# Turning the gated stage's x in 32x32 squares on VectorE instead of on TensorE

## The chip, the cores and the metric

The kernel runs on one core of one Trainium2 chip. The metric is the device time of one execution in microseconds; the kernel before takes 614.62 us (median of three runs).

## The reference

Three layers follow one another: a recurrent attention over 4 x 8 heads of 768 steps, a mixture of eight experts over its 3072 tokens of 384 features, and the gated layers. The change touches the last alone, where N is 3072, DM 384 and FM 1024:

```python
def _moe2_ref(x, w1, w2, w3, w_out) -> np.ndarray:
    a = x @ w1
    b = x @ w2
    h = a * b @ w3
    return (h @ w_out).astype(np.float32)
```

## The kernel before

The core's engines run their own instruction streams and meet at semaphores. The attention comes first (to about 120 us), then routing and the experts, whose output rows are scattered to `xbuf` in DRAM, then `gated_layers` from about 300 us on. The product w3 @ w_out is folded into one matrix `wf` ahead of it (`Fold`), with TensorE's last part of that work placed around the first block.

`gated_layers` cuts the 3072 tokens into NB = 6 blocks of TOK = 512 (NI = 4 tiles of 128 tokens). A block needs x with its features on the partitions: KD = 3 tiles of 128 features by 512 tokens. Each float32 operand is split into a part `hi` that float32r holds and the remainder `lo`, and a product is made of three matmuls, hi by hi, hi by lo and lo by hi.

- SyncE (`gx.load`, L1082) loads a block's 512 rows of `xbuf` into `x_in`, tokens on the partitions, in two transfers of 384 KB; `x_in` has two slots, in the memory of an expert's weights that are no longer needed. The loads of blocks 0 and 1 are issued at the end of the experts, when the last scatter has landed; load(n) waits for TensorE's transposes of block n-2 (semaphore `s_T`). Its queue also issues the stores of the output (L1472), in the order load(n+2), store(n).
- TensorE turns x by 12 transposes of 128x128 a block (`transposes`, L1496), 8 into the banks `p_ab[0]` and 4 into a bank of `p_ab[1]`, and those of block n+1 stand at the end of block n. Then, for each of the KF = 8 tiles f of 128 hidden features, come `gates(t, f)` (L1508; 18 matmuls of 128x512, for a and b) and `outputs(t, f - 1)` (L1523; 12 matmuls of 128x384 that accumulate in the banks `p_o`).
- ScalarE makes `xT_hi` from PSUM (L1573), and per f copies a to SBUF (L1565, `a_sb`) and splits g into `g_hi` (L1568).
- VectorE makes `xT_lo` from PSUM (L1595), and per f the product g = a * b (L1588, `g_sb`) and `g_lo` (L1590).
- At the end of a block both copy `p_o` to `o_sb` (`out_copy`, L1579 and L1601), and SyncE stores it.

The order is written out by hand, engine by engine; `rounds` unrolls the first and last two blocks and loops over the two in the middle. `gates(t, f)` waits for g of f-2 (its banks), `outputs(t, f)` for `g_lo` of f, `outputs(t, 0)` also for the output copies of the block before. At the end of a block TensorE's order is gates(7), eight transposes of the next block, outputs(6), four transposes, outputs(7), and then gates(0) and gates(1) of the next block with nothing between them.

Of the kernel before, what the change touches and what calls it, by code (L numbers as in the profile page):

```python
# [12 lines left out]
P = 128  # L13
# [19 lines left out]

LINE = 1024
FRONT = 128
TABLE_BYTES = 2656


# [1030 lines left out]
class GatedInputs:  # L1069
# [3 lines left out]
    def __init__(self, sem, w1_in, TOK, DM):  # L1073
        self.TOK = TOK
        self.x_in = [w1_in[:, :, :].rearrange("p k f -> p (k f)")[:, i * TOK // P * DM:(i + 1) * TOK // P * DM].rearrange("p (i d) -> p i d", d=DM)
                     for i in range(2)]
        self.s_x = [[sem(f"x{i}{h}") for h in range(2)] for i in range(2)]

    def load(self, sp, xbuf, slot, n):
        TOK = self.TOK  # L1080
        for h in range(2):
            sp.dma_start(self.x_in[slot][:, 2 * h:2 * h + 2, :],  # L1082
                         xbuf[bass.ds(n * TOK + h * TOK // 2, TOK // 2), :].rearrange("(i p) d -> p i d", p=P)).then_inc(self.s_x[slot][h], 16)


def experts(nc, env, w1, w2, xbuf):
# [9 lines left out]
    with ExitStack() as ctx:  # L1096
# [74 lines left out]
        @block.sync  # L1171
        def _(sp):
            def load_w1(t, e=None):
                wait(sp, s_w1lo, t.num(NG, 0))
                ex.load_w1(sp, t.num() if e is None else e)

            def load_w2(t, e=None):
                wait(sp, s_w2lo, t.num(NG, 0))
                ex.load_w2(sp, t.num() if e is None else e)
            def load_wm(t):  # L1180
                if wm_block(t):
                    return
                wait(sp, fold.s_T, fold.KF)
                wait(sp, s_wmlo, t.num(1, -1))
                sp.dma_start(fold.w3_in[t.slot][:, :], wm[t.slot][bass.ds(t.turn(P), P), :]).then_inc(s_wmin[t.slot], 16)
            n = count_over(sp)
            sp.wait_ge(s_x[0], 32)
            rounds(sp, whole(sp, (load_wm, 0), (load_w1, 1), (load_w2, 1)), 2, E, 0, 0)

            def body(t, o):  # L1190
                e = sp.value_load(env["over_expert"][0:1, bass.ds(o, 1)], min_val=0, max_val=E - 1)
                load_w1(t, e)
                load_w2(t, e)
            overflow(sp, body, n)
            sp.wait_ge(s_w1lo, E * NG)
            sp.wait_ge(s_over, 1)
            for s in s_out:
                sp.wait_ge(s, 32 * env["n_scattered"])
            for i in range(2):
                env["gated_x"].load(sp, xbuf, i, i)  # L1200

        @block.gpsimd
        def _(pool):
# [207 lines left out]
def gated_layers(nc, env, xbuf, out):  # L1411
# [7 lines left out]
    with ExitStack() as ctx:  # L1419
# [3 lines left out]
        def sem(name):  # L1423
            return ctx.enter_context(nc.semaphore("gl_" + name))
# [9 lines left out]
        g_lo = [sb(f"g_lo{i}", [P, TOK], F32R) for i in range(2)]  # L1434
        o_sb = [sb(f"o_sb{i}", [P, NI, DM]) for i in range(2)]
        gx = env["gated_x"]
        x_in, s_x = gx.x_in, gx.s_x
        s_T, s_xhi, s_xlo = sem("T"), sem("xhi"), sem("xlo")
        s_ab, s_a, s_g, s_ghi, s_glo = sem("ab"), sem("a"), sem("g"), sem("ghi"), sem("glo")
        s_gout, s_o, s_oact, s_odve = sem("gout"), sem("o"), sem("oact"), sem("odve")  # L1440
        s_st = [sem(f"st{i}") for i in range(2)]
# [17 lines left out]
        with nc.Block() as block:  # L1459
            @block.sync  # L1460
            def _(sp):
                def load(t):
                    if isinstance(t.c, int) and t.num() < 2:
                        return
                    wait(sp, s_T, t.num(2, -2))
                    gx.load(sp, xbuf, t.slot, t.num())

                def store(t):
                    for h in range(2):
                        wait(sp, s_oact, t.num(2, h + 1))  # L1470
                        wait(sp, s_odve, t.num(2, h + 1))
                        sp.dma_start(out[bass.ds(t.num(TOK, h * TOK // 2), TOK // 2), :].rearrange("(i p) d -> p i d", p=P),  # L1472
                                     o_sb[t.slot][:, 2 * h:2 * h + 2, :]).then_inc(s_st[t.slot], 16)
                rounds(sp, whole((load, 2), (store, 0)), 2, NB, 2, 0)
                for i in range(2):
                    sp.wait_ge(s_st[i], 32 * NB // 2)
# [8 lines left out]
            def _(pe):  # L1485
                fold.product(pe, KF - 1, p_o[-1], (2,))
                pe.wait_ge(env["s_wmlo"], 2 * KD)

                def transposes(t, part):

                    wait(pe, s_g, t.num(KF, part - 1))
                    for i in range(NI):
                        if part == 0 and i % 2 == 0:
                            wait(pe, s_x[t.slot][i // 2], t.turn(16, 16))
                        for k in ((0, 1), (2,))[part]:
                            m = pe.transpose(p_ab[part][k % 2][:, i * P:(i + 1) * P], x_in[t.slot][:, i, k * P:(k + 1) * P], ident[:, :])  # L1496
                    m.then_inc(s_T, 1)

                def gates(t, f):
                    if f >= 2:  # L1500
                        wait(pe, s_g, t.num(KF, f - 1))
                    cols = slice(f * P, (f + 1) * P)
                    for w in range(2):
                        for k in range(KD):
# [22 lines left out]
                    m.then_inc(s_gout, 1)  # L1527

                def step(c, j):
                    t, nxt = Item(c, j, 0, 2), Item(c, j, 1, 2)  # L1530
                    if t.inside(NB):
                        for f in range(KF):
                            gates(t, f)
                            if f == KF - 1 and nxt.inside(NB):
                                transposes(nxt, 0)
                            if f:
                                outputs(t, f - 1)
                    if nxt.inside(NB):
                        if not t.inside(NB):
                            transposes(nxt, 0)  # L1540
                        transposes(nxt, 1)
                        if not t.inside(NB):
                            fold.product(pe, KF - 1, p_o[-1], (3,))
                    if t.inside(NB):
                        outputs(t, KF - 1)
                rounds(pe, step, 2, NB, 1, 0)

            @block.scalar
            def _(act):
# [1 line left out]
                    act.wait_ge(fold.s_Wout, f + 1)  # L1551
                    act.activation(wf_hi[:, f, :], fold.wf[:, f, :], ACT.Copy).then_inc(s_wfhi, 1)

                def wf_parts(t):

                    if isinstance(t.num(), int) and t.num() == 0:
                        for f in range(KF):
                            if f == KF - 1:
                                fold.taken(act, f, p_o[-1])
                            wf_part(f)  # L1560

                def products(t):
                    for f in range(KF):
                        wait(act, s_ab, t.num(KF, f + 1))
                        act.activation(a_sb[f % 2][:, :], p_ab[f % 2][0][:, :], ACT.Copy).then_inc(s_a, 1)  # L1565
                        wait(act, s_g, t.num(KF, f + 1))
                        wait(act, s_gout, t.num(KF, f - 1))
                        act.activation(g_hi[f % 2][:, :], g_sb[f % 2][:, :], ACT.Copy).then_inc(s_ghi, 1)  # L1568

                def x_hi(t):  # L1570
                    for k in range(KD):
                        wait(act, s_T, t.num(2, 1 + k // 2))
                        act.activation(xT_hi[t.slot][:, k, :], p_ab[k // 2][k % 2][:, :], ACT.Copy).then_inc(s_xhi, 1)  # L1573

                def out_copy(t):
                    wait(act, s_st[t.slot], t.turn(32))
                    for i in range(0, NI, 2):
                        first_or_all(act, t, i)
                        act.activation(o_sb[t.slot][:, i, :], p_o[i][:, 0:DM], ACT.Copy).then_inc(s_oact, 1)  # L1579
                rounds(act, whole((products, 0), (x_hi, 1), (wf_parts, 1), (out_copy, 0)), 2, NB, 1, 0)  # L1580

            @block.vector
            def _(dve):
                def products(t):
                    for f in range(KF):
                        wait(dve, s_a, t.num(KF, f + 1))
                        wait(dve, s_glo, t.num(KF, f - 1))
                        dve.tensor_tensor(g_sb[f % 2][:, :], a_sb[f % 2][:, :], p_ab[f % 2][1][:, :], ALU.mult).then_inc(s_g, 1)  # L1588
                        wait(dve, s_ghi, t.num(KF, f + 1))
                        dve.tensor_tensor(g_lo[f % 2][:, :], g_sb[f % 2][:, :], g_hi[f % 2][:, :], ALU.subtract).then_inc(s_glo, 1)  # L1590

                def x_lo(t):
                    for k in range(KD):
                        wait(dve, s_xhi, t.num(KD, k + 1))
                        dve.tensor_tensor(xT_lo[t.slot][:, k, :], p_ab[k // 2][k % 2][:, :], xT_hi[t.slot][:, k, :], ALU.subtract).then_inc(s_xlo, 1)  # L1595

                def out_copy(t):
                    wait(dve, s_st[t.slot], t.turn(32))
                    for i in range(1, NI, 2):
                        first_or_all(dve, t, i)  # L1600
                        dve.tensor_copy(o_sb[t.slot][:, i, :], p_o[i][:, 0:DM]).then_inc(s_odve, 1)  # L1601
                rounds(dve, whole((products, 0), (x_lo, 1), (out_copy, 0)), 2, NB, 1, 0)


def program(nc, r, k, v, w, u, moe_w_skip, moe_w_gate, moe_w1, moe_w2, moe2_w1, moe2_w2, moe2_w3, moe2_w_out, out):
# [83 lines left out]
```

## Time and profile before

| | us |
|---|---|
| median of three runs | 614.62 (613.81 to 615.62) |
| span of the profiled execution | 612.5 |
| around the span, against the median | 2.1 |
| TensorE busy in it | 595.1 (97%) |
| VectorE, ScalarE, GpSimd busy | 286.4, 228.1, 156.5 |

The profiled execution has no time of its own beside its span; the difference of 2.1 us to the median stands for what lies around it. A span goes from the first to the last instruction. PE is TensorE's matmuls, PEld its weight loads, DVE VectorE, ACT ScalarE, POOL GpSimd, SP SyncE, and SPq the transfers that it issues. PEclk is the clock that TensorE was granted, as a share of its full speed. Matmuls are pipelined, so that their recorded durations overlap: what one costs is read from the distance to the next start.

### The profile page before, as it was taken

How to read it: one execution, taken by the hardware profiler on the slowest of the kernel's cores; microseconds unless marked ns; L12 is line 12 of the kernel's file. 1: busy time of each engine (PE TensorE's matmuls, PEld its weight loads, DVE VectorE, ACT ScalarE, POOL GpSimd, SP SyncE). 2: the span in 40 equal slices, each digit the busy share in tenths (PEclk: the TensorE clock that was granted, in tenths of full speed). 3: DMA queues.
4: the chain of work that ended last, by engine and by line, in shares of the span. 5: the costliest groups of instructions: out<-in, count | busy, mean ns of one | idle time of the engine just before them, and what ended most of it. 6: DMA issues, size and time to landing. Idle time of an engine off the chain costs nothing.

```text
span 612.5 us, 17307 instructions
## 1 busy us (share of the span) xinstructions
PE 595.1 (97%) x7355; PEld 532.3 (87%) x7355; DVE 286.4 (47%) x459; ACT 228.1 (37%) x410; POOL 156.5 (26%) x179
## 2 busy tenths in 40 slices
PE   6699999999999999999999999999999999999997
PEld 6699999766999999999688888888898888888886
DVE  5489889283777777774121332232132133223212
ACT  3156666444665555552321222132132122213212
POOL 7568887215055544441230000000000000000000
PEclk9899999999999999999999999999999999999999
DMA  7779997596566777630400030020011001001001
GB/s 130 133 145 187 188 184 188 206 313 241 181 237 246 277 274 271 237 130 20 164 1 0 1 103 1 1 103 1 0 57 48 1 1 51 1 1 51 1 0 52
DMA packets 104258, 67.80 MB, mean 111 GB/s; under 512 B 79708, under 2 KB 98272, under 8 KB 104216
## 3 DMA queue, kind: packets, MB, share of 16 engines
q1 hardware_dynamic: 76360, 57.91, 30.8%
q10 hardware_dynamic: 25552, 4.72, 4.1%
q0 software_dynamic: 2304, 4.59, 2.3%
q8 instruction: 29, 0.48, 0.3%
q14 instruction: 13, 0.11, 0.1%
HBM read 55.92 MB, written 12.20 MB: 111 GB/s over the span
## 4 chain that ended last, share of the span: by engine, by line
PE 50%; DVE 0%; ACT 0%; issue 0%
PE gl_pab L1508 32%; PE gl_po L1523 8%; PE p_pair L1523 8%; PE gl_pab L1496 1%; PE p_pair L93 0%; DVE gl_g_lo L1590 0%; DVE gl_g_sb L1588 0%; ACT gl_g_hi L1568 0%; ACT gl_a_sb L1565 0%; DVE gl_o_sb L1601 0%
## 5 line engine op out<-in xcount | busy, mean ns | idle before, releaser
L1588 DVE TENSOR_TENSOR gl_g_sb<-gl_a_sb,gl_pab 128x512 f32<-128x512 f32 x48 | 33.0, 688 | 186.3 <-ACT gl_a_sb L1565 186.3
L1508 PE MATMUL gl_pab<-gl_xT_hi,wm_lo 128*128 128x512 f32 x288 | 112.9, 392 | 0.0
L1508 PE MATMUL gl_pab<-gl_xT_lo,wm_hi 128*128 128x512 f32 x288 | 112.8, 392 | 0.0
L1508 PE MATMUL gl_pab<-gl_xT_hi,wm_hi 128*128 128x512 f32 x288 | 112.1, 389 | 0.0
L1565 ACT ACTIVATE gl_a_sb<-gl_pab 128x512 f32<-128x512 f32 x48 | 28.8, 599 | 183.9 <-PE gl_pab L1508 183.9
L1508 PEld LDWEIGHTS gl_pab<-gl_xT_hi,wm_lo 128*128 128x128 f32 x288 | 54.0, 188 | 11.4
L1508 PEld LDWEIGHTS gl_pab<-gl_xT_hi,wm_hi 128*128 128x128 f32 x288 | 54.1, 188 | 10.6 <-DVE gl_xT_lo L1595 0.3
L1508 PEld LDWEIGHTS gl_pab<-gl_xT_lo,wm_hi 128*128 128x128 f32 x288 | 54.0, 188 | 10.5
L1265 PE MATMUL ex_ph<-ex_xT_hi,ew_w_hi 128*128 128x224 f32 x192 | 52.9, 275 | 0.0
L1265 PE MATMUL ex_ph<-ex_xT_hi,ew_w_lo 128*128 128x224 f32 x192 | 52.7, 274 | 0.0
L1265 PE MATMUL ex_ph<-ex_xT_lo,ew_w_hi 128*128 128x224 f32 x192 | 52.7, 274 | 0.0
L1590 DVE TENSOR_TENSOR gl_g_lo<-gl_g_sb,gl_g_hi 128x512 fp32r<-128x512 f32 x48 | 33.2, 692 | 33.5 <-ACT gl_g_hi L1568 33.5
L1568 ACT ACTIVATE gl_g_hi<-gl_g_sb 128x512 fp32r<-128x512 f32 x48 | 30.3, 632 | 36.2 <-DVE gl_g_sb L1588 36.2
L1281 PE MATMUL p_pair<-ew_w_hi,ex_h_hi 128*96 128x384 f32 (+1 forms) x128 | 43.4, 339 | 0.0
L1281 PE MATMUL p_pair<-ew_w_hi,ex_h_lo 128*96 128x384 f32 (+1 forms) x128 | 43.0, 336 | 0.0
L1281 PE MATMUL p_pair<-ew_w_lo,ex_h_hi 128*96 128x384 f32 (+1 forms) x128 | 43.0, 336 | 0.0
L1042 POOL DMA_INDIRECT ew_x_in<-xbuf,slot_token x16 | 22.5, 1406 | 71.3 <-DVE ex_x_new L1392 50.3
L93 PE MATMUL p_pair<-wo,w3T 128*128 128x384 f32 x112 | 38.8, 489 | 0.5 <-PEq L1652 0.4
L1265 PEld LDWEIGHTS ex_ph<-ex_xT_hi,ew_w_hi 128*128 128x128 f32 x192 | 36.8, 192 | 0.2
L1265 PEld LDWEIGHTS ex_ph<-ex_xT_lo,ew_w_hi 128*128 128x128 f32 x192 | 36.8, 192 | 0.1
L1265 PEld LDWEIGHTS ex_ph<-ex_xT_hi,ew_w_lo 128*128 128x128 f32 x192 | 36.9, 192 | 0.0
L1523 PE MATMUL gl_po<-gl_wf_hi,gl_g_hi 128*128 128x384 f32 x96 | 33.5, 349 | 0.7 <-DVE gl_g_lo L1590 0.7
(197 smaller groups left out, 1223.3 us busy)
## 6 DMA issues: line engine op xcount, KB each, us to landing
w_in<-in_moe_w SPq DMA_DIRECT2D x8, 1536.0 KB
ew_w_in<-in_moe_w SPq DMA_DIRECT2D x8, 1536.0 KB
w_in<-in_moe_w SPq DMA_DIRECT2D x14, 512.0 KB, 9.4
k_in<-in_k SPq DMA_DIRECT2D x48, 96.0 KB
v_in<-in_v ACTq DMA_DIRECT2D x48, 96.0 KB, 3.5
r_in<-in_r SPq DMA_DIRECT2D x48, 96.0 KB
w_in<-xbuf SPq DMA_DIRECT2D x12, 384.0 KB, 4.1
out<-gl_o_sb SPq DMA_DIRECT2D x12, 384.0 KB, 2.4
```

Of the source, the lines that this page charges most:

```text
L93: m = pe.matmul(bank[:, 0:self.DM], self.w3T[i % 3][:, g, :], self.wo[:, g, :], start=(g == 0), stop=(g == self.KF - 1), skip_group_check= ...
L1042: pool.indirect_dma_start(self.x_in[slot][0:tokens.shape[0], i, :], None, xbuf[:, :], bass.IndirectOffsetOnAxis(ap=tokens, axis=0), bounds ...
L1265: m = pe.matmul(p_h[g][:, f % 2, 0:width(t)], a[:, k, cols], b[:, k, 0:width(t)], start=(k == 0 and n == 0), stop=(k == KD - 1 and n == 2))
L1281: m = pe.matmul(p_y[i][0:n_tok, 0:DM], a[:, f, cols], b[:, f, :], start=(f == 0 and n == 0), stop=(f == KF - 1 and n == 2))
L1496: m = pe.transpose(p_ab[part][k % 2][:, i * P:(i + 1) * P], x_in[t.slot][:, i, k * P:(k + 1) * P], ident[:, :])
L1508: m = pe.matmul(p_ab[f % 2][w][:, :], a[:, w * KD + k, cols], b[t.slot][:, k, :], start=(k == 0 and n == 0), stop=(k == KD - 1 and n == 2))
L1523: m = pe.matmul(p_o[i][:, 0:DM], a[f % 2][:, cols], b[:, f, :], start=(f == 0 and n == 0), stop=(f == KF - 1 and n == 2))
L1565: act.activation(a_sb[f % 2][:, :], p_ab[f % 2][0][:, :], ACT.Copy).then_inc(s_a, 1)
L1568: act.activation(g_hi[f % 2][:, :], g_sb[f % 2][:, :], ACT.Copy).then_inc(s_ghi, 1)
L1588: dve.tensor_tensor(g_sb[f % 2][:, :], a_sb[f % 2][:, :], p_ab[f % 2][1][:, :], ALU.mult).then_inc(s_g, 1)
L1590: dve.tensor_tensor(g_lo[f % 2][:, :], g_sb[f % 2][:, :], g_hi[f % 2][:, :], ALU.subtract).then_inc(s_glo, 1)
```

## The change

Block 0 is loaded and turned as before (`load_first`, `first_transposes`). For blocks 1 to 5, the load writes x into `x_quad`, a view of the same two slots, in twelve transfers. Partition quarter q takes, of each tile k of 128 features, the 32 features k * 128 + 32 q to + 31: on its partition t lie, for each group g of 32 tokens, the features of token 32 g + t. VectorE then turns the 32x32 squares of one k by one instruction (`x_turn`, 128x512) into a new tile `xT`, with the features on the partitions. x_hi and x_lo of these blocks read `xT` instead of PSUM. All this is done in the steps of the block before: x_turn(k) in f = 1 + k, x_hi(k) in f = 2 + k, x_lo(k) in f = 3 + k.

TensorE's transposes of blocks 1 to 5 go, and its order becomes one sequence over the blocks: gates(0) of the next block comes ahead of outputs(7) of the block before it, and the output copies come behind the product of f = 0 of the next block. load(n) for n over 2 waits for the turns of block n-2 (`s_turned`).

```diff
+        self.x_quad = [x.rearrange("p i d -> p (i d)").rearrange("p (g k e) -> p g k e", k=DM // P, e=QUAD) for x in self.x_in]
+        self.s_x = [sem(f"x{h}") for h in range(2)]
+        self.s_xq = [sem(f"xq{i}") for i in range(2)]
...
+    def load(self, sp, xbuf, slot, n):
+        TOK = self.TOK
+        rows = xbuf[bass.ds(n * TOK, TOK), :].rearrange("(g t) (k q e) -> q k t g e", t=QUAD, q=P // QUAD, e=QUAD)
+        for q in range(P // QUAD):
+            for k in range(self.x_quad[slot].shape[2]):
+                sp.dma_start(self.x_quad[slot][q * QUAD:(q + 1) * QUAD, :, k, :], rows[q, k]).then_inc(self.s_xq[slot], 16)
...
-            for i in range(2):
-                env["gated_x"].load(sp, xbuf, i, i)
+            env["gated_x"].load_first(sp, xbuf)
+            env["gated_x"].load(sp, xbuf, 1, 1)
...
+        xT = sb("xT", [P, KD, TOK])
+        NQ = 16 * KD * P // QUAD
+        s_T, s_turned, s_xhi, s_xlo = sem("T"), sem("turned"), sem("xhi"), sem("xlo")
...
-                    wait(sp, s_T, t.num(2, -2))
+                    if isinstance(t.c, int) and t.num() == 2:
+                        sp.wait_ge(s_T, 2)
+                    else:
+                        wait(sp, s_turned, t.num(KD, -2 * KD))
...
-                    if f >= 2:
-                        wait(pe, s_g, t.num(KF, f - 1))
+                    wait(pe, s_g, t.num(KF, f - 1))
...
-                    t, nxt = Item(c, j, 0, 2), Item(c, j, 1, 2)
-                    if t.inside(NB):
-                        for f in range(KF):
+                    t, before = Item(c, j, 0, 2), Item(c, j, -1, 2)
+                    for f in range(KF):
+                        if t.inside(NB):
                             gates(t, f)
-                            if f == KF - 1 and nxt.inside(NB):
-                                transposes(nxt, 0)
-                            if f:
+                        if f:
+                            if t.inside(NB):
                                 outputs(t, f - 1)
-                    if nxt.inside(NB):
-                        if not t.inside(NB):
-                            transposes(nxt, 0)
-                        transposes(nxt, 1)
-                        if not t.inside(NB):
-                            fold.product(pe, KF - 1, p_o[-1], (3,))
-                    if t.inside(NB):
-                        outputs(t, KF - 1)
-                rounds(pe, step, 2, NB, 1, 0)
+                        elif before.inside(NB):
+                            outputs(before, KF - 1)
+                first_transposes(0)
+                first_transposes(1)
+                fold.product(pe, KF - 1, p_o[-1], (3,))
+                rounds(pe, step, 2, NB, 0, 1)
...
+                def x_hi(t, k):
+                    wait(act, s_turned, t.num(KD, k + 1 - KD))
+                    act.activation(xT_hi[t.slot][:, k, :], xT[:, k, :], ACT.Copy).then_inc(s_xhi, 1)
...
+                def step(c, j):
+                    t, before, nxt = Item(c, j, 0, 2), Item(c, j, -1, 2), Item(c, j, 1, 2)
+                    for f in range(KF):
+                        if t.inside(NB):
+                            product(t, f)
+                        if f == 0 and before.inside(NB):
+                            out_copy(before)
+                        if 2 <= f < 2 + KD and nxt.inside(NB):
+                            x_hi(nxt, f - 2)
...
+                def x_turn(t, k):
+                    if k == 0:
+                        wait(dve, s_xq[t.slot], t.turn(NQ, NQ if t.slot else 0))
+                    wait(dve, s_xlo, t.num(KD, k + 1 - KD))
+                    dve.transpose(xT[:, k, :].rearrange("p (g e) -> p g e", e=QUAD), x_quad[t.slot][:, :, k, :]).then_inc(s_turned, 1)
+                def x_lo(t, k):
+                    wait(dve, s_xhi, t.num(KD, k + 1))
+                    dve.tensor_tensor(xT_lo[t.slot][:, k, :], xT[:, k, :], xT_hi[t.slot][:, k, :], ALU.subtract).then_inc(s_xlo, 1)
...
+                def step(c, j):
+                    t, before, nxt = Item(c, j, 0, 2), Item(c, j, -1, 2), Item(c, j, 1, 2)
+                    for f in range(KF):
+                        if t.inside(NB):
+                            product(t, f)
+                        if f == 0 and before.inside(NB):
+                            out_copy(before)
+                        if nxt.inside(NB):
+                            if 1 <= f < 1 + KD:
+                                x_turn(nxt, f - 1)
+                            if 3 <= f < 3 + KD:
+                                x_lo(nxt, f - 3)
```

## Rows read from the trace of the kernel before

**Rows 1.** The page's part 1: busy us (share of the span) and number of instructions.

```profile
PE 595.1 (97%) x7355; PEld 532.3 (87%) x7355; DVE 286.4 (47%) x459; ACT 228.1 (37%) x410; POOL 156.5 (26%) x179
```

**Rows 2.** Windows, one block each: busy us (instructions), granted clock, DMA share, GB/s.

```profile
455.90:507.00 51.10, 51.10 (x254) 45.11 (x253) 13.95 (x21) 12.40 (x21) 0.00 (x0) 1.00 0.10 32
507.00:558.00 51.00, 51.00 (x254) 45.01 (x253) 13.96 (x21) 12.40 (x21) 0.00 (x0) 1.00 0.04 16
```

**Rows 3.** The chain that ended last, in order of time (start, us, engine, line).

```profile
568.56 4.12 PE gl_pab L1508 x18
```

**Rows 4.** Windows of the transposes' line L1496 alone, one block.

```profile
404.80:455.90 51.10, 1.63 (x12) 1.43 (x12) 1.00 0.09 32
```

**Rows 5.** Timeline of ACT: start, us, line, tile, shapes, idle before it and releaser.

```profile
311.13 0.60 ACT L1565 ACTIVATE gl_a_sb<-gl_pab 128x512 f32<-128x512 f32 x1 [2.10 <-PE gl_pab L1508]
...
362.20 0.60 ACT L1565 ACTIVATE gl_a_sb<-gl_pab 128x512 f32<-128x512 f32 x1 [2.10 <-PE gl_pab L1508]
...
399.57 0.60 ACT L1565 ACTIVATE gl_a_sb<-gl_pab 128x512 f32<-128x512 f32 x1 [4.24 <-PE gl_pab L1508]
...
413.27 0.60 ACT L1565 ACTIVATE gl_a_sb<-gl_pab 128x512 f32<-128x512 f32 x1 [2.10 <-PE gl_pab L1508]
...
603.86 0.60 ACT L1565 ACTIVATE gl_a_sb<-gl_pab 128x512 f32<-128x512 f32 x1 [4.24 <-PE gl_pab L1508]
```

**Rows 6.** Timeline of PE at the end of block 1, and in block 5.

```profile
399.13 0.39 PE L1508 MATMUL gl_pab<-gl_xT_hi,wm_lo 128*128 128x512 f32 x1
...
400.16 0.42 PE L1523 MATMUL gl_po<-gl_wf_hi,gl_g_hi 128*128 128x384 f32 x1
...
402.18 0.34 PE L1523 MATMUL p_pair<-gl_wf_hi,gl_g_lo 128*128 128x384 f32 x1
...
402.70 0.42 PE L1523 MATMUL gl_po<-gl_wf_hi,gl_g_hi 128*128 128x384 f32 x1
...
597.20 0.39 PE L1508 MATMUL gl_pab<-gl_xT_hi,wm_lo 128*128 128x512 f32 x1
597.43 0.33 PE L1523 MATMUL gl_po<-gl_wf_hi,gl_g_hi 128*128 128x384 f32 x1
597.60 0.34 PE L1523 MATMUL gl_po<-gl_wf_lo,gl_g_hi 128*128 128x384 f32 x1
```

**Rows 7.** Timeline of DVE and PE in block 0, f=1 and 2.

```profile
313.15 0.69 DVE L1590 TENSOR_TENSOR gl_g_lo<-gl_g_sb,gl_g_hi 128x512 fp32r<-128x512 f32 x1 [0.70 <-ACT gl_g_hi L1568]
317.99 0.69 DVE L1588 TENSOR_TENSOR gl_g_sb<-gl_a_sb,gl_pab 128x512 f32<-128x512 f32 x1 [4.14 <-ACT gl_a_sb L1565]
319.37 0.69 DVE L1590 TENSOR_TENSOR gl_g_lo<-gl_g_sb,gl_g_hi 128x512 fp32r<-128x512 f32 x1 [0.70 <-ACT gl_g_hi L1568]
...
323.38 0.33 PE L1523 MATMUL gl_po<-gl_wf_hi,gl_g_hi 128*128 128x384 f32 x1
```

**Rows 8.** DVE: L1601 (ns min/median/max), L536 (busy us, mean ns); ACT: L1568 likewise.

```profile
L1601 DVE COPY gl_o_sb<-p_pair x6: 557/558/558, 354.0 to 609.0; 128x384 f32<-128x384 f32 x6
...
L536 DVE TENSOR_TENSOR w_sq<-w_sq 128x4 f32<-128x4 f32 x6 | 1.0, 161 | 0.2
...
L1568 ACT ACTIVATE gl_g_hi<-gl_g_sb 128x512 fp32r<-128x512 f32 x48 | 30.3, 632 | 36.2 <-DVE gl_g_sb L1588 36.2
```

**Rows 9.** DMA of 1 to 26 us by queue; issue durations of L262; landings, page part 6.

```profile
q1 hardware_dynamic: 14990, 2.79, 59.4%
...
L262 SPq DMA_DIRECT2D k_in<-in_k x48: 595/638/1684, 1.7 to 93.1; - x48
...
v_in<-in_v ACTq DMA_DIRECT2D x48, 96.0 KB, 3.5
...
w_in<-xbuf SPq DMA_DIRECT2D x12, 384.0 KB, 4.1
```

**Rows 10.** Timeline of SP's transfers and of PE at the stage's start.

```profile
294.74 7.76 SPq L1082 DMA_DIRECT2D w_in<-xbuf  x6
...
300.12 1.15 PE L1496 MATMUL gl_pab<-ident,w_in 128*128 128x128 f32 x9
```

More of the change, by code:

```diff
@@ L35 @@
 FRONT = 128
+QUAD = 32
 TABLE_BYTES = 2656
@@ L1076, in __init__, with load_first @@
                      for i in range(2)]
-        self.s_x = [[sem(f"x{i}{h}") for h in range(2)] for i in range(2)]
+        self.x_quad = [x.rearrange("p i d -> p (i d)").rearrange("p (g k e) -> p g k e", k=DM // P, e=QUAD) for x in self.x_in]
+        self.s_x = [sem(f"x{h}") for h in range(2)]
+        self.s_xq = [sem(f"xq{i}") for i in range(2)]
+    def load_first(self, sp, xbuf):
+        TOK = self.TOK
+        for h in range(2):
+            sp.dma_start(self.x_in[0][:, 2 * h:2 * h + 2, :],
+                         xbuf[h * TOK // 2:(h + 1) * TOK // 2, :].rearrange("(i p) d -> p i d", p=P)).then_inc(self.s_x[h], 16)
     def load(self, sp, xbuf, slot, n):
         TOK = self.TOK
-        for h in range(2):
-            sp.dma_start(self.x_in[slot][:, 2 * h:2 * h + 2, :],
-                         xbuf[bass.ds(n * TOK + h * TOK // 2, TOK // 2), :].rearrange("(i p) d -> p i d", p=P)).then_inc(self.s_x[slot][h], 16)
+        rows = xbuf[bass.ds(n * TOK, TOK), :].rearrange("(g t) (k q e) -> q k t g e", t=QUAD, q=P // QUAD, e=QUAD)
+        for q in range(P // QUAD):
+            for k in range(self.x_quad[slot].shape[2]):
+                sp.dma_start(self.x_quad[slot][q * QUAD:(q + 1) * QUAD, :, k, :], rows[q, k]).then_inc(self.s_xq[slot], 16)
 def experts(nc, env, w1, w2, xbuf):
@@ L1436, in gated_layers @@
         gx = env["gated_x"]
-        x_in, s_x = gx.x_in, gx.s_x
-        s_T, s_xhi, s_xlo = sem("T"), sem("xhi"), sem("xlo")
+        x_in, s_x, x_quad, s_xq = gx.x_in, gx.s_x, gx.x_quad, gx.s_xq
+        xT = sb("xT", [P, KD, TOK])
+        NQ = 16 * KD * P // QUAD
+        s_T, s_turned, s_xhi, s_xlo = sem("T"), sem("turned"), sem("xhi"), sem("xlo")
         s_ab, s_a, s_g, s_ghi, s_glo = sem("ab"), sem("a"), sem("g"), sem("ghi"), sem("glo")
@@ L1487, in _, with first_transposes @@
                 pe.wait_ge(env["s_wmlo"], 2 * KD)
-                def transposes(t, part):
-                    wait(pe, s_g, t.num(KF, part - 1))
+                def first_transposes(part):
                     for i in range(NI):
                         if part == 0 and i % 2 == 0:
-                            wait(pe, s_x[t.slot][i // 2], t.turn(16, 16))
+                            pe.wait_ge(s_x[i // 2], 16)
                         for k in ((0, 1), (2,))[part]:
-                            m = pe.transpose(p_ab[part][k % 2][:, i * P:(i + 1) * P], x_in[t.slot][:, i, k * P:(k + 1) * P], ident[:, :])
+                            m = pe.transpose(p_ab[part][k % 2][:, i * P:(i + 1) * P], x_in[0][:, i, k * P:(k + 1) * P], ident[:, :])
                     m.then_inc(s_T, 1)
                 def gates(t, f):
-                    if f >= 2:
-                        wait(pe, s_g, t.num(KF, f - 1))
+                    wait(pe, s_g, t.num(KF, f - 1))
                     cols = slice(f * P, (f + 1) * P)
@@ L1552, in wf_part, with wf_parts, product, first_x_hi @@
                     act.activation(wf_hi[:, f, :], fold.wf[:, f, :], ACT.Copy).then_inc(s_wfhi, 1)
[L1554 to L1562, printed above, removed]
-                    for f in range(KF):
[L1564 to L1570, printed above, removed]
-                    for k in range(KD):
-                        wait(act, s_T, t.num(2, 1 + k // 2))
-                        act.activation(xT_hi[t.slot][:, k, :], p_ab[k // 2][k % 2][:, :], ACT.Copy).then_inc(s_xhi, 1)
+                def wf_parts():
+                    for f in range(KF):
+                        if f == KF - 1:
+                            fold.taken(act, f, p_o[-1])
+                        wf_part(f)
+                def product(t, f):
+                    wait(act, s_ab, t.num(KF, f + 1))
+                    act.activation(a_sb[f % 2][:, :], p_ab[f % 2][0][:, :], ACT.Copy).then_inc(s_a, 1)
+                    wait(act, s_g, t.num(KF, f + 1))
+                    wait(act, s_gout, t.num(KF, f - 1))
+                    act.activation(g_hi[f % 2][:, :], g_sb[f % 2][:, :], ACT.Copy).then_inc(s_ghi, 1)
+                def first_x_hi():
+                    for k in range(KD):
+                        act.wait_ge(s_T, 1 + k // 2)
+                        act.activation(xT_hi[0][:, k, :], p_ab[k // 2][k % 2][:, :], ACT.Copy).then_inc(s_xhi, 1)
+                def x_hi(t, k):
+                    wait(act, s_turned, t.num(KD, k + 1 - KD))
+                    act.activation(xT_hi[t.slot][:, k, :], xT[:, k, :], ACT.Copy).then_inc(s_xhi, 1)
                 def out_copy(t):
@@ L1579, in out_copy @@
                         act.activation(o_sb[t.slot][:, i, :], p_o[i][:, 0:DM], ACT.Copy).then_inc(s_oact, 1)
-                rounds(act, whole((products, 0), (x_hi, 1), (wf_parts, 1), (out_copy, 0)), 2, NB, 1, 0)
+                def step(c, j):
[7 more added lines that the diff above has]
+                            x_hi(nxt, f - 2)
@@ L1582, in _ @@
+                first_x_hi()
+                wf_parts()
+                rounds(act, step, 2, NB, 0, 1)
             @block.vector
             def _(dve):
[L1584 to L1590, printed above, removed]
@@ L1592, in x_lo, with product @@
-                def x_lo(t):
-                    for k in range(KD):
-                        wait(dve, s_xhi, t.num(KD, k + 1))
-                        dve.tensor_tensor(xT_lo[t.slot][:, k, :], p_ab[k // 2][k % 2][:, :], xT_hi[t.slot][:, k, :], ALU.subtract).then_inc(s_xlo, 1)
+                def product(t, f):
+                    wait(dve, s_a, t.num(KF, f + 1))
+                    wait(dve, s_glo, t.num(KF, f - 1))
+                    dve.tensor_tensor(g_sb[f % 2][:, :], a_sb[f % 2][:, :], p_ab[f % 2][1][:, :], ALU.mult).then_inc(s_g, 1)
+                    wait(dve, s_ghi, t.num(KF, f + 1))
+                    dve.tensor_tensor(g_lo[f % 2][:, :], g_sb[f % 2][:, :], g_hi[f % 2][:, :], ALU.subtract).then_inc(s_glo, 1)
@@ new lines, in first_x_lo @@
+                def first_x_lo():
+                    for k in range(KD):
+                        dve.wait_ge(s_xhi, k + 1)
+                        dve.tensor_tensor(xT_lo[0][:, k, :], p_ab[k // 2][k % 2][:, :], xT_hi[0][:, k, :], ALU.subtract).then_inc(s_xlo, 1)
+                def x_turn(t, k):
[3 more added lines that the diff above has]
+                    dve.transpose(xT[:, k, :].rearrange("p (g e) -> p g e", e=QUAD), x_quad[t.slot][:, :, k, :]).then_inc(s_turned, 1)
@@ L1601, in out_copy @@
                         dve.tensor_copy(o_sb[t.slot][:, i, :], p_o[i][:, 0:DM]).then_inc(s_odve, 1)
-                rounds(dve, whole((products, 0), (x_lo, 1), (out_copy, 0)), 2, NB, 1, 0)
+                def step(c, j):
[10 more added lines that the diff above has]
+                                x_lo(nxt, f - 3)
+                first_x_lo()
+                rounds(dve, step, 2, NB, 0, 1)
 def program(nc, r, k, v, w, u, moe_w_skip, moe_w_gate, moe_w1, moe_w2, moe2_w1, moe2_w2, moe2_w3, moe2_w_out, out):
```

## Prediction

> **What bounds the kernel now.** I read the page's busy shares first: TensorE is busy for 97% of the span [rows 1], and the gated stage, which starts near 300 us [rows 10], is half of it. The reader is to see next that this stage has no other limit: cut into its six blocks, every window of a full block shows PE busy for its whole length at a granted clock of 1.00, with DVE at 14.0 us and ACT at 12.4 us of 51 [rows 2]. The chain of waits says the same: it runs through PE's matmuls, in pieces like the 18 of a gates group in 4.12 us [rows 3]. So an instruction of PE that goes away in blocks 0 to 4 is worth its whole slot, as long as nothing else becomes late; work moved to DVE costs nothing while it fits DVE's idle time. The slots are read from the starts of consecutive instructions, not from the durations, because the pipelined matmuls overlap: the 12 transposes of one block count as 1.63 us busy [rows 4], but take less, as follows.
>
> **What is removed: the transposes of blocks 1 to 5 on PE, 60 of them.** ScalarE starts each a_sb copy as soon as a gates group ends, so its starts are the clock of the stage. Inside a block, from f=1 to f=7, they are 399.57 - 362.20 = 37.37 us apart, 6.228 us per step (18 gates matmuls, 12 outputs matmuls) [rows 5]. From f=7 of one block to f=1 of the next it is 413.27 - 399.57 = 13.70 us, where two plain steps would be 12.46: the block boundary costs 1.24 us. After the change a boundary is a plain step: PE does gates(0) of the new block, then outputs(7) of the old one. Over the stage: from f=1 of block 0 (311.13) to f=7 of block 5 (603.86) is 292.73 us [rows 5]; there are 46 steps, and 46 x 6.228 = 286.49. **Saved: 6.24 us.** The other way to size it is the gap that the transposes open: last gates matmul to first outputs matmul 1.03 us with the first eight between them, 0.23 without; the last four sit in a gap of 0.52 us where 0.17 is usual [rows 6]. That is 0.80 + 0.35 = 1.15 us, and up to 0.09 more for each of the two outputs groups behind a transpose, whose first matmul lasts 0.42 us instead of 0.33: at most 1.33 us a block, 6.65 us in all. I take 6.24, since it is measured over the whole stage, with all that a boundary does to the matmuls around it, and keep 6.65 for the low end.
>
> **What is added on DVE: three turns of 128x512 a block**, in steps f=1 to 3, and x_lo in f=3 to 5. DVE is idle 4.14 us in front of the g_sb of a step [rows 7]. No row shows a 32x32 transpose. From below, a DVE copy of 384 columns is 0.56 us [rows 8]. From above, if each of the 16 squares of a row were paid like an instruction of its own, the row of a tiny DVE instruction, 0.161 us [rows 8], gives 2.6 us. I take 0.7, as a pass over 128x512 is 0.69 us [rows 7] and the number of elements is the same. The fullest step is f=3: one turn and one x_lo, 1.4 of 4.1 us. At 2.6 it still fits (3.3). Behind it stands a second cover: g_lo of f=2 is done at 319.37 + 0.69 = 320.06 and PE takes it up at 323.38, 3.3 us later [rows 7]. So PE waits only once three turns together pass 3 x 4.14 - 0.69 + 3.3 = 15.0 us, 5.0 each. Cost: nothing. The Trainium skill ("VectorE: DVE Perf Modes", The three transpose paths) sends a 128x128 transpose to TensorE, since DVE only turns 32x32 squares; here the load brings the quarters into place, and by that page's 311 ns for 128x128 in bf16 the turn would be an estimated four times that at most, 1.2 us, which changes nothing in the sum.
>
> **What moves on ACT and DVE.** The three x_hi and x_lo leave the boundary, where they read PSUM, and go into steps with 4.1 to 4.2 us idle; a pass over SBUF costs 0.63 us on ACT (g_hi) [rows 8] and 0.69 on DVE (g_lo) [rows 7]: nothing. x_hi(k) waits for a turn that was made a step earlier, and behind it on ACT stands only the next a_sb. The output copies now lie behind product(0) of the next block, and outputs(0), one gates group later, waits for them. With T the end of gates(0): g_lo ends at T + 2.7 (the distance from ACT's a_sb at 311.13 to the end of g_lo at 313.84), the two DVE copies of 0.56 us follow [rows 8] and end at T + 3.9; PE needs them at T + 6.2, a whole step later (outputs, 2.1, then gates, 4.1). Cover 2.3 us: nothing. If it failed it would cost PE its excess at each of five boundaries.
>
> **What moves on SP and the DMA queues.** A load was 2 issues of 384 KB and becomes 12 of 64 KB, 512 packets of 128 bytes each. The nearest rows are k_in and r_in: 96 KB, also 512 packets (192 bytes), 0.638 us an issue; and the queue that carried them moved 14990 packets in 25 us in 59.4% of 16 engines' time, 16 ns a packet [rows 9]. So 32 packets per engine take 0.5 us, less than the issue: SP sets the pace, 12 x 0.64 = 7.7 us a load. Block 0's own load keeps its form and goes first. Block 1's starts about 1 us after SP's first issue at 294.74 and is all issued by 303.5; with the 3.5 us from issue to landing of the v_in row [rows 9] it is there by 307. DVE asks for it after g_lo of f=1, at 313.84; 7 us to spare, and PE itself would not wait before 317.99 - 0.7 + 3.3 = 320.6 [rows 7, 10]. Block 2's load (303.5 to 311.2) has until block 1. Loads 3 to 5 come behind a store, as before, and in front of the next store, a block of 51 us later [rows 2]; each has over 40 us. A new wait stands on SP: load(n) on the turns of block n-2, made a whole block before. Cost: nothing. That loads don't slow PE shows in two blocks, one with a load under it (DMA share 0.10) and one without (0.04): PE does the same 254 matmuls in both in 51.1 and 51.0 us [rows 2].
>
> What stays: block 0's start, the fold, the last outputs, copies and stores. Block 0's load may land a little earlier or later now that smaller packets stand behind it: plus or minus 0.4 us, estimated from its 5.4 us between 294.74 and the transposes at 300.12 [rows 10].
>
> **Sum.** The profiled span is 612.5 us, and the runs' median 614.62, 2.1 us around it. Span after: 606.3; time: 614.62 - 6.24 = **608.4 us**.
>
> **Rivals.**
> (a) *Block 1's load lands too late, slower than before.* Transfers into a quarter of the partitions may be slower than into half. DVE then stands at x_turn with g_sb of f=2 behind it, ACT and PE follow. It begins to cost at 320.6, that is if each of the 12 transfers takes over (320.6 - 295.8)/12 = 2.1 us, 3.2 times the row's 0.64; it reaches slower than before at 2.6 us each. At 3 us, 295.8 + 36 = 332, a stall of 11: 620 us. Only the first load can, unless a load takes over 50 us. Against it: the rows' packets go to half of the partitions at 16 ns each, and the new ones keep 32 elements in order on both sides. Chance 0.04. The Trainium skill ("VectorE: DVE Perf Modes", The three transpose paths) speaks for this rival: a plain copy that transposes by its strides is 19 times slower than one through the crossbar. By it a load would take an estimated 19 x 4.1 us [rows 9] = 78 us, over a block, all five would bound, and the time would pass 680 us; no row shows such a copy. The same notes speak against it ("SBUF — State Buffer", Door 1: The DMA port swizzle): a range of 32 partitions reaches as many ports as one of 64.
> (b) *A turn over 5 us.* Each us above it costs PE 3 us a block, 15 us in all; slower than before from 5.4 us. Three turns of 6 us: 608.4 + 15 = 623. For it: no row shows the operation. Against: even 16 separate instructions stay below, at 2.6 us. Chance 0.02.
> (c) *The gain is given back at the boundary:* outputs(0) waits for the output copies, or gates(1) for the last g. The rows leave 2.3 us of cover, so it would take an order on ACT or DVE that I misread. With 1.2 us of wait per boundary: 614.4, no change. Chance 0.05.
> (d) *PE's pace falls,* because DVE, ACT and DMA now read and write beside matmuls at more places. 0.5% of 292 us is 1.5: 609.9; against it stand the equal blocks of [rows 2]. Chance 0.05.
> Forecast as it stands, 0.84.
>
> **How the numbers follow.** Low: lowest run 613.81 - 6.65 - 0.4 = 606.8. High: highest run 615.62 - 6.24 = 609.4, plus one unseen wait of 0.4 us at each of five boundaries, 611.4; that takes in (d). About 0.3%, 1.8 us, is what a measurement of this kernel can tell from no change. Faster: forecast and most of (d), 0.89. Same: (c) and the rest, 0.05. Slower: (a) and (b), 0.06.
>
> **What would show it.** In the profile after: 12 PE transposes instead of 72, all ahead of block 0; a_sb starts 6.23 us apart across the boundaries too; no PE idle with DVE as its releaser; a DVE group of 15 turns near 0.7 us; DVE's wait in front of the first turn empty; the load's issues near 0.64 us. I would be wrong if PE shows idle time near 314 to 330 us (a), DVE fills its steps (b), PE waits at the boundaries (c), or a step is longer than 6.23 us (d).

## Result and profile after

The changed kernel takes 616.42 us (median of 20 runs, 613.97 to 618.61) against 615.05 us for the kernel before in the same comparison: a ratio of 1.0021, 95% interval 1.0012 to 1.0030. It is slower by 0.2%, where 608.4 us were forecast. The profiled execution is the fastest of the 20, 613.97 us with a span of 612.2, which is 0.3 us under the span of the kernel before (612.5).

The page's part 1 of the kernel after, to be held against [rows 1]: the sixty transposes are gone (7355 to 7295 PE instructions), DVE has 15 more.

```profile
PE 590.4 (96%) x7295; PEld 526.9 (86%) x7295; DVE 294.7 (48%) x474; ACT 227.0 (37%) x410; POOL 156.4 (26%) x179
```

Inside the stage everything went as forecast. The timeline of ACT after, f=1 of block 0 and f=7 of block 5, answers to [rows 5]; under it the durations of the turns (min/median/max, ns):

```profile
317.12 0.60 ACT L1575 ACTIVATE gl_a_sb<-gl_pab 128x512 f32<-128x512 f32 x1 [2.09 <-PE gl_pab L1524]
...
603.55 0.60 ACT L1575 ACTIVATE gl_a_sb<-gl_pab 128x512 f32<-128x512 f32 x1 [4.24 <-PE gl_pab L1524]
...
L1627 DVE STREAM_TRANSPOSE gl_xT<-w_in x15: 703/705/705, 319.7 to 531.5; 128x512 f32<-128x512 f32 x15
```

286.43 us lie between the two copies, 6.30 less than before; forecast were 286.49 and 6.24. A turn costs 0.70 us. But the first line stands at 317.12 where it stood at 311.13: the stage begins 6.0 us later. The timelines of SP and PE after show where, beside [rows 10]:

```profile
294.99 0.93 SPq L1086 DMA_DIRECT2D w_in<-xbuf  x2
295.97 6.85 SPq L1096 DMA_DIRECT2D w_in<-xbuf  x12
...
295.86 2.74 PE L94 MATMUL p_pair<-wo,w3T 128*128 128x384 f32 x8
...
303.35 2.90 PE L94 MATMUL p_pair<-wo,w3T 128*128 128x384 f32 x4 [4.75 <-PEq L1702]
306.04 1.56 PE L1513 MATMUL gl_pab<-ident,w_in 128*128 128x128 f32 x12
```

PE finishes its part of the fold at 298.6 and stands 4.75 us. Its releaser is no tile but L1702, the line `with nc.Block(no_gpsimd_drain=True) as block:` (PEq is TensorE's sequencer). That line encloses attention, routing and experts, and at its end the engines meet: the traces show it here for PE and SP, and below for ACT. SP comes there only when it has issued the last of its fourteen transfers, at 302.8; PE goes on 0.5 us later. The kernel before has the same meeting point. Its waits (engine, waited for: us, times, longest) and its PE timeline show it:

```profile
SPq L1652 <- PEq L1652: 1.3, 1, 1.3
...
PE p_pair L93 <- PEq L1652: 0.4, 1, 0.4
...
298.76 1.53 PE L93 MATMUL p_pair<-wo,w3T 128*128 128x384 f32 x4 [0.41 <-PEq L1652]
```

There SP had issued four transfers by 297.1, and PE came last, at 298.4, so that SP's issues held up nobody. The second loss follows from the first. Windows of the kernel after (PE, PEld, DVE, ACT and POOL busy with instructions, then granted clock, DMA share, GB/s):

```profile
300.00:302.00 2.00, 0.00 (x0) 0.00 (x0) 0.00 (x0) 0.00 (x0) 0.00 (x0) 1.00 0.80 125
302.00:304.00 2.00, 0.65 (x1) 0.50 (x2) 0.00 (x0) 0.00 (x0) 0.00 (x0) 0.70 0.78 123
304.00:306.00 2.00, 2.00 (x4) 0.89 (x3) 0.00 (x0) 0.00 (x0) 0.00 (x0) 0.50 0.08 14
306.00:308.00 2.00, 2.00 (x15) 1.78 (x14) 0.17 (x1) 0.80 (x2) 0.00 (x0) 0.95 0.00 0
```

While PE is idle its clock falls from 1.00 to 0.50 (1.2 of 2.4 GHz); the windows put the low stretch at 302.8 to 306.2. The fold's next four matmuls take 303.35 to 306.04, 2.69 us, where the kernel before needs 1.36 (298.76 to the transposes at 300.12 [rows 10]): 1.3 us more. The twelve transposes behind them take 1.40 instead of 1.31, another 0.1. Together: 4.6 (the next matmul starts at 303.35 instead of 298.76) + 1.4 = 6.0 us.

### The profile page after: what moved, and what is told of

Read it like the earlier page. It is cut to its first block and busy times, and to the rows that moved or that the text cites. A ratio compares the mean times of both kernels' runs of the same rounds, so it can differ in the third digit from the quotient of the medians.

```text
span 612.2 us, 17257 instructions
## 1 busy us (share of the span) xinstructions
PE 590.4 (96%) x7295; PEld 526.9 (86%) x7295; DVE 294.7 (48%) x474; ACT 227.0 (37%) x410; POOL 156.4 (26%) x179
## 5 line engine op out<-in xcount | busy, mean ns | idle before, releaser
L94 PE MATMUL p_pair<-wo,w3T 128*128 128x384 f32 x112 | 40.2, 503 | 4.9 <-PEq L1702 4.7
L94 PEld LDWEIGHTS p_pair<-wo,w3T 128*128 128x128 f32 x112 | 20.7, 195 | 17.3 <-issue 5.9
```

What stands on the lines that cost most here:

```text
L94: m = pe.matmul(bank[:, 0:self.DM], self.w3T[i % 3][:, g, :], self.wo[:, g, :], start=(g == 0), stop=(g == self.KF - 1), skip_group_check= ...
```

## Experiments

Theory B: the meeting point is held by SP's issues, and the clock falls behind PE's idle time. Rival P: the small packets themselves delay block 0's data or PE. Rival L: the load is late for VectorE. Every time stands beside runs of the kernel before on the same chip (medians 615.20, 614.68 and 614.56).

**Block 1's load behind the meeting point.** The line leaves `experts` and opens SP's part of `gated_layers`:

```diff
-            env["gated_x"].load(sp, xbuf, 1, 1)
...
+                gx.load(sp, xbuf, 1, 1)
                 rounds(sp, whole((load, 2), (store, 0)), 2, NB, 2, 0)
```

> Block 1's load in twelve transfers is issued by SyncE behind the end of the experts' block of code instead of ahead of it; all else is the changed kernel. Theory B (the end of that block is a meeting point of all engines, SyncE reaches it only when it has issued its last transfer, TensorE stands 4.7 us, and its clock then falls): TensorE's wait at the meeting point is back near 0.4 us, its clock stays at 1.00 there, the whole predicted 6.2 us show: 608 to 609 us. Rival P (the small packets of block 1's load delay block 0's own data or what else TensorE needs): the packets come 3 us later and still beside block 0's start; part of the loss stays, over 611 us. Rival L (the load is now too late for VectorE's first turn): a gap on VectorE behind the g_lo of f=1 in block 0, and TensorE idle near 320 us.

Measured: 608.86 us, ratio 0.9891 (0.9874 to 0.9907). PE's wait at the meeting point, from this kernel's waits, is that of the kernel before:

```profile
PE p_pair L94 <- PEq L1702: 0.4, 1, 0.4
```

SP issues from 300.73 on, and the first turn starts at 315.77, directly behind the g_lo of f=1, with no wait for the load. The packets now fall into block 0's start and cost nothing there: from f=1 of block 0 to f=7 of block 5 it is 286.43 us again. B holds; P and L fall. This version is 1.1% below the kernel before, and its median lies below the changed kernel's 616.42.

**Six of the twelve behind.** The load of block 1 is split by partition quarters, two ahead and two behind.

> Six of block 1's twelve transfers ahead of the end of the experts' block of code, six behind it. Theory B: each transfer ahead costs what SyncE takes to issue it, 0.5 to 0.6 us; with six fewer TensorE's wait is shorter by 3 to 3.6 us, 1.1 to 1.7 us instead of 4.7, and the time lies between the changed kernel and the one with all twelve behind: 610 to 612 us. Rival P: the time follows the packets in flight, not the issues, and stays within 1 us of the changed kernel.

Measured: 612.42 us, ratio 0.9948 (0.9931 to 0.9965). PE waits:

```profile
PE p_pair L94 <- PEq L1702: 3.0, 1, 3.0
```

The time is 0.4 us above the expected 610 to 612, and the wait is longer than the expected 1.1 to 1.7: SP needed until 301.0, 0.8 us for each of the six. Its timeline shows that four of them took 0.5 us and two 1.25 and 1.39 us. The two long ones stand between 297.8 and 300.5, where block 0's data are moving (DMA share 1.04 from 298 to 300); that this makes them long is not shown. In this profile the clock did not fall.

**The kernel before, with block 1's load in twelve pieces.** TensorE turns it as ever, packets are 512 bytes:

```diff
...
+        for i in range(4):
+            for k in range(3):
+                sp.dma_start(self.x_in[1][:, i, k * P:(k + 1) * P],
+                             xbuf[TOK + i * P:TOK + (i + 1) * P, k * P:(k + 1) * P]).then_inc(self.s_first, 16)
```

> The kernel before with nothing changed but block 1's load: twelve transfers of 128 rows by 128 features (64 KB each, packets of 512 bytes) instead of two of 384 KB; TensorE still turns it. Theory B: twelve issues hold the end of the experts' block of code as in the changed kernel, TensorE waits 4 to 5 us there, its clock falls, and the time is 5 to 7 us over the kernel before, 620 to 622 us. Rival P: 512-byte packets are a quarter in number, so block 0's data come as in the kernel before: within 1 us of it. If only the gap and not the clock costs: 619 us.

Measured: 621.81 us, ratio 1.0106 (1.0090 to 1.0123). The clock fell to 0.50 here too. Its waits and SP's timeline:

```profile
PE p_pair L93 <- PEq L1665: 3.8, 1, 3.8
...
295.80 5.69 SPq L1092 DMA_DIRECT2D w_in<-xbuf  x12
```

Neither small packets nor VectorE's turns are needed for the loss: twelve issues ahead of the meeting point make it, 6.6 us in the medians. The profile is that of the fastest run (619.22); its span is 4.9 us over that of the kernel before, 3.4 of it the longer wait and 1.5 the clock.

**TensorE kept busy.** A call of the kernel's helper `keep_warm` at the end of TensorE's experts' code, with 60 and then with 40 transposes of the identity, whose result is unused:

```diff
             fold.product(pe, KF - 1, p_y[1], (0, 1))
+            keep_warm(pe, ident, p_h[3][:, 0, :], 60)
```

> The changed kernel with 60 transposes of the identity (128x128, about 0.1 us each, their result is unused) at the end of TensorE's experts' code, ahead of the meeting point that it waits at. The wait becomes work of about 5.8 us, so TensorE may come 1 us late itself. Theory B with its clock part: the clock does not fall to 0.5 at 304 to 306 us, the four matmuls of the fold take 1.5 us instead of 2.9, and the time is 1 to 2.5 us below the changed kernel: 614 to 615.5 us. If the clock has no part in it: the changed kernel's time or up to 1 us above, 616.5 to 617.5 us.

> As the run with 60 transposes of the identity ahead of the meeting point, but 40, 0.112 us each, 4.5 us: TensorE's idle time becomes work and TensorE doesn't come late. The meeting point stays where SyncE's issues put it, near 303.3 us; the clock should stay at 1.00. Theory B with the clock part: the wait itself (4.3 us over that of the kernel with the load behind) still costs and only the clock's part goes: 608.9 + 4.3 = 613.2 us, 612.7 to 614. Without the clock part: 616.4 us.

Measured: 615.18 us (ratio 0.9997, 0.9987 to 1.0007) and 613.83 us (0.9989, 0.9977 to 1.0000). With 60, TensorE came 2 us late itself (at 305.4, SP's last issue ending at 303.0), and the time still fell below the changed kernel's 616.4. With 40 it is 2.2 us below the changed kernel in the same comparison (616.06), with the clock at 1.00 from 298 to 310. Part of these 2.2 us is the clock (1.4 to 1.5 by the two profiles of the changed kernel); a chance difference in SP's issue time can be the rest, which is not shown. Some 5 us over the version with the load behind stay, and that is the meeting point alone: between the end of the fold's part and the next matmul of the fold lie 5.7 us here and 0.4 there.

**The changed kernel again.**

> The changed kernel as it is, for a second profile and beside the others on one chip. Its first profile (span 612.2 us, mean clock 0.992) was 2.4 us under its median. Theory B with the clock part: the typical run spends longer at the lower clock behind TensorE's idle time at the meeting point; a profile near the median shows the same wait of 4 to 5.5 us and a granted clock under 1.00 for more than the 2 us of the first one, and the time is 616 to 617 us. Rival: the clock is lower elsewhere (in the attention), and the stage's start looks like the first profile's.

Measured: 616.06 us, ratio 1.0021 (1.0006 to 1.0036), as the first time. The new profile has a span of 615.3; its waits and windows:

```profile
PE p_pair L94 <- PEq L1702: 6.2, 1, 6.2
...
302.00:304.00 2.00, 0.00 (x0) 0.00 (x0) 0.00 (x0) 0.00 (x0) 0.00 (x0) 0.65 0.58 87
304.00:306.00 2.00, 0.00 (x0) 0.00 (x0) 0.00 (x0) 0.00 (x0) 0.00 (x0) 0.50 0.82 128
306.00:308.00 2.00, 1.68 (x3) 1.10 (x4) 0.00 (x0) 0.00 (x0) 0.00 (x0) 0.50 0.44 71
308.00:310.00 2.00, 2.00 (x10) 1.29 (x10) 0.00 (x0) 0.00 (x0) 0.00 (x0) 0.64 0.00 0
```

The wait is 6.2 us instead of 4.75, where 4 to 5.5 was expected: SP's twelve issues took from 298.10 to about 305.8, 0.64 us each instead of 0.57. The fold's four matmuls take 2.69 us again, the twelve transposes 1.5 instead of 1.3. So the clock costs 1.5 us here, little more than in the first profile. My expectation that a typical run spends longer at the low clock was right: the stretch reaches from 302.6 to 309.4, twice as long. What it implied, that this costs more, was wrong, since TensorE stood idle in the first 3.7 us of it. Of the 3.1 us between the two spans 1.5 are the wait and 1.5 lie ahead of it: SP's first issue comes at 296.48 instead of 294.99, and the mean clock of the first 100 us is 0.93 instead of 0.97. The rival is right in that half. The same happens to other kernels: in the version with the load behind, that issue comes at 296.73.

**VectorE's cover.** In the version with the load behind, every turn is made six, then ten times, the further ones into spare tiles (shown for six; with ten, nine go into seven spare tiles and the reuse of two waits for a semaphore):

```diff
+                    for i in range(5):
+                        dve.transpose(spare[i][:, :].rearrange("p (g e) -> p g e", e=QUAD), x_quad[t.slot][:, :, k, :])
                     dve.transpose(xT[:, k, :].rearrange("p (g e) -> p g e", e=QUAD), x_quad[t.slot][:, :, k, :]).then_inc(s_turned, 1)
```

> The kernel with block 1's load behind, in which VectorE makes each turn six times (five into spare tiles that nobody reads). The prediction's cover: 4.14 us idle a step on VectorE, and 3.3 us until TensorE needs g_lo. Six turns start about 0.63 us apart, 3.8 us in steps f=1 and 2, 4.4 with x_lo in f=3: 0.3 us over the idle time, inside the second cover. Expected: the time of the kernel with the load behind, 608.9 us, within 0.8 us. If the work of VectorE cost TensorE anything (shared memory, rival d) 75 more turns would show it: 1 us or more above.

> The same with each turn made ten times (nine into spare tiles). Three steps take 3 x 6.3 + 0.6 = 19.5 us where the two covers hold 12.4 + 3.3 = 15.7: TensorE waits 3.8 us in each of five blocks, 19 us, 628 us, with VectorE's g_lo as the releaser of outputs in f=3; more if the clock falls behind the gaps. If the covers were wrongly read: below 622 or above 634 us.

Measured: 607.85 us (ratio 0.9886, 0.9869 to 0.9902) and 625.80 us (1.0191, 1.0170 to 1.0213). Seventy-five more turns cost nothing (the median is 1.0 us below the version with the load behind, where 0.8 to either side was expected), the step stays at 6.23 us, and rival (d) falls as far as VectorE's work goes. With ten the time is 16.9 us over the version with the load behind (608.86), 3.4 a block, where 3.8 were expected. The releaser is the expected one, by the waits of the run with ten:

```profile
PE gl_po L1541 <- DVE gl_g_lo L1617: 10.2, 5, 2.0
```

The five waits of 2.0 us are not the whole price. By the starts of the a_sb copies the five blocks in which turns are made lose 2.5, 4.1, 2.5, 4.1 and 2.5 us, 15.7 in all. In the second and the fourth the clock fell to 0.50 (392.7 to 396.1 and 498.5 to 501.9), 1.4 and 1.0 us after TensorE had started again; there the loss is 1.6 us larger. Behind the other three waits, as long to 0.02 us, the clock stayed at 1.00.

**Control: the kernel before with its two transfers behind.**

> The kernel before with its two transfers of block 1 moved behind the meeting point, as a control: what the move alone is worth. In the kernel before SyncE has issued its four transfers by 297.1 us and TensorE comes to the meeting point at 298.4, so SyncE does not hold it: within 0.8 us of the kernel before. If the move alone gained 2 us or more, the 6.3 us of the kernel with the turns on VectorE and the load behind would not be the transposes'.

Measured: 614.38 us, ratio 1.0000 (0.9992 to 1.0009). The move alone is worth nothing where SP doesn't hold the meeting point.

**Two queues.** The changed kernel, quarters 0 and 1 issued by SP, 2 and 3 by ACT, all ahead of the meeting point.

> The changed kernel with block 1's twelve transfers all ahead of the meeting point, six issued by SyncE and six by ScalarE, which waits for the same semaphores and has nothing else to do there. If what holds the meeting point is each engine's own time to issue: TensorE's wait falls to about the 3.0 us of the run with six ahead, 611.5 to 613 us. If it is how fast the transfers are taken by the shared DMA engines (512 small packets each): the wait stays near 4.7 us or more, 615 to 617 us.

Measured: 611.39 us, ratio 0.9950 (0.9935 to 0.9965), 0.1 us below the range expected if issuing sets the pace. Its waits, the issues of both, PE and a window:

```profile
PE p_pair L94 <- PEq L1706: 2.3, 1, 2.3
...
295.87 3.80 SPq L1095 DMA_DIRECT2D w_in<-xbuf  x6
296.62 3.70 ACTq L1095 DMA_DIRECT2D w_in<-xbuf  x6
...
300.83 2.45 PE L94 MATMUL p_pair<-wo,w3T 128*128 128x384 f32 x4 [2.29 <-PEq L1706]
...
300.00:302.00 2.00, 1.17 (x3) 0.76 (x4) 0.00 (x0) 0.00 (x0) 0.00 (x0) 0.82 1.38 214
```

Both queues issue side by side, at 0.63 and 0.62 us each, and the packets flow at 214 GB/s where the changed kernel has 125 between 300 and 302. SP has issued its last at 299.7 and ACT at 300.3, and PE goes on 0.5 us behind ACT: what holds the meeting point is the time of the engine that issues longest. The Trainium skill ("DMA: Bandwidth & Descriptors", Rules for kernel authors) says that spreading transfers over queues brings no bandwidth and only saves issue time; the saved issue time is what this run shows, and since issuing was the limit the rate rose with it. The clock fell to 0.50 behind only 2.3 us of idle time here, at 301.3, when TensorE had been working again for 0.5 us; it did not fall behind 3.0 us in the run with six behind.

## Why the prediction was wrong

**The step that failed** stands under what moves on SP and the DMA queues: "Block 1's starts about 1 us after SP's first issue at 294.74 and is all issued by 303.5", followed by "Cost: nothing". The number was right (302.8). The question who waits for SP to have issued was asked for the data and for what is queued behind on SP, not for the end of the block of code in which the issues stand. The rows to see it were there: PE's 0.4 us wait with L1652 as its releaser, and SP's 1.3 us on the same line, just ahead of block 0. With them, and with what the clock turned out to cost, the step would have read: PE arrives at 298.4, SP at 303.5, 5 us of wait and up to 1.5 us of clock behind it; 608.4 + 5 to 6.5 = 613.4 to 614.9 us, no change. None of my rivals had this mechanism; (a) looked at the same transfers, but for their landing. They landed in 2.4 us in the median, 3.5 at most, so that nothing of the 19-fold price which (a) weighs shows in them.

**The size of it.** Against the version with the load behind, the changed kernel's median is 7.6 us higher (616.42 - 608.86, from two comparisons). The two profiles give 4.3 of wait + 1.4 of clock = 5.7 and 5.8 + 1.5 = 7.3 us; the first is that of the fastest run, the second that of a run 1 us over its median. The kernel before had only 0.4 us at that place, so the loss outweighs the 6.2 us gained by 1.4.

**What held.** The saving on PE: 6.24 forecast, 6.30 in the profile; the version with the load behind gives 608.86, 0.5 above the forecast and inside its range. The turn: 0.7 forecast, 0.70 measured, against bounds of 0.56 and 2.6. VectorE's two covers: six turns are free, ten cost 16.9 us against 19. The output copies and the x_hi and x_lo: no PE wait at any boundary. The landing: with the load 5 us later than in the changed kernel it is still in time. Rivals (b), (c) and (d) didn't occur; of (a), only that the time would be lost at the first load.

**The issue price.** The forecast's 0.64 us came from k_in; loads 3 to 5 run at 0.57 (6.83 us for twelve), those at the stage's start at 0.54 to 0.8. Nearly all single issues last 0.46 to 0.49 us with the next 0.53 us behind their start; what differs is one or two ahead of the meeting point that last 0.98 to 1.70 us and start between 297.8 and 301.0. In the kernel before with twelve pieces (128 packets each instead of 512) none lasts over 0.46 us. Why the long ones are long stays open.

## What to carry to other kernels

Splitting a transfer into many costs the issuing engine time, 0.5 to 0.8 us each here, and that time is free only if nobody waits for the engine itself: look for the next point at which all engines meet, and for waits whose releaser is a line instead of a tile, however short they are now. Put long runs of issues behind such a point if their data can wait. If TensorE must stand there anyway, count its clock too.

## What the runs showed of the hardware

The meeting point: where the issuing engine came last, TensorE went on 0.51 to 0.53 us after the last issue had ended (the changed kernel twice, the runs with six behind, twelve pieces, 40 transposes and two queues); where TensorE came last, 0.41 to 0.43 us after its own work (the kernel before, and the runs with the load behind, 60 transposes and the two transfers behind).

TensorE's clock behind an idle stretch: it stayed at 1.00 after 0.4, 1.3 and 3.0 us, and fell to 0.50 after 2.3, 3.8, 4.7 and 6.2 us; of five waits of 2.0 us in one run it fell behind two. The length alone does not decide it. It fell while TensorE was still idle (both profiles of the changed kernel) or 0.5 to 1.4 us after it had started again. Between TensorE's start behind the meeting point and the first gates matmul lie 3.8 us at 1.00 (six profiles), and 5.2, 5.3, 5.4 and 5.5 us where it fell: 1.4 to 1.7 us each time.

A 32x32 turn of 128x512 in float32 takes 0.70 us on VectorE, and ten in a row start 0.60 us apart. Seventy-five more of them left TensorE's step at 6.23 us.
